# Four PSUM places for the transposes and one pair for the scores in the first batch of an attention and MLP kernel

## What is computed

```python
# attention, B, H, S, D = 4, 8, 576, 64
scores = causal_mask(q @ k.T / sqrt(D))
a = exp(scores - scores.max(-1)); a /= a.sum(-1) + 1e-9
phi = lambda x: where(x > 0, x, exp(x) - 1) + 1
mem = (phi(q) @ M_prev) / (phi(q) @ z_prev + 1e-6)
g = sigmoid(beta)                       # one gate for each head
x = g * mem + (1 - g) * (a @ v)         # 2304 tokens x 512
# first MLP, 512 -> 2048 -> 512
h = x @ w_in; y = (h * sigmoid(h)) @ w_out
# second MLP, 512 -> 1024 -> 512
h = y @ w2_in; u = h * softmax(h)
out = layer_norm(u) * g_ln @ w2_out
```

## Time and profile before

| | us |
|---|---|
| median of 3 runs | 880.93 |
| lowest and highest | 878.12, 881.41 |
| the profiled execution | 878.63 |
| its span, first to last instruction | 876.8 |

### The profile page before, as it was taken

The page is one execution under the profiler, slowest core; times in us unless marked ns, Lnnn a source line. Parts: engine busy times, 40 slices in busy tenths (PEclk is TensorE's granted clock), DMA queues, the critical chain, the costliest instruction groups (busy, mean ns, idle before and its releaser), DMA issues.

```text
span 876.8 us, 13106 instructions
## 1 busy us (share of the span) xinstructions
PE 834.5 (95%) x4576; PEld 702.8 (80%) x4576; DVE 524.0 (60%) x1003; ACT 405.3 (46%) x897; POOL 327.3 (37%) x350
## 2 busy tenths in 40 slices
PE   3868799999999999999999999999999999999998
PEld 2656677888788887878888879999998888888886
DVE  4787675876775576675575543144426666666664
ACT  3686676666655555565555434334121222222222
POOL 3667657677644455455544314133110000000000
PEclk9996789999999999999999999999999999999999
DMA  5222247657775454554444347333300000000000
GB/s 174 60 86 59 75 129 241 219 200 225 229 238 170 151 176 145 168 158 152 150 155 154 122 143 306 126 121 125 138 3 12 14 24 24 24 24 24 24 13 37
DMA packets 67480, 105.63 MB, mean 120 GB/s; under 512 B 29024, under 2 KB 40288, under 8 KB 67168
## 3 DMA queue, kind: packets, MB, share of 16 engines
q1 hardware_dynamic: 67120, 104.85, 36.7%
q10 hardware_dynamic: 304, 0.05, 0.0%
HBM read 83.38 MB, written 21.50 MB: 120 GB/s over the span
## 4 chain that ended last, share of the span: by engine, by line
PE 75%; DVE 5%; DMA 5%; SPq 4%; POOL 4%; ACT 4%; issue 2%; ACTq 0%
PE banks L1344 19%; PE banks L1332 18%; PE banks L1402 11%; PE banks L1463 11%; PE banks L1287 4%; PE banks L1309 4%; DMA wr_raw<-in_w_out 2%; PE banks L1249 2%; PE banks L1452 2%; SPq L493 2%; DMA z_row<-in_z_prev 1%; POOL vm L629 1%; PE banks L1303 1%; DVE pt_lo L984 1%; POOL g_lo L641 1%
## 5 line engine op out<-in xcount | busy, mean ns | idle before, releaser
L1344 PE MATMUL banks<-g_hi,wr 128*128 128x512 f32 (+1 forms) x640 | 197.2, 376 | 3.2 <-POOL g_lo L641 1.9
L624 POOL TENSOR_SCALAR prob<-prob,inv_sum,gate_all 128x576 f32<-128x576 f32 (+2 forms) x144 | 95.5, 674 | 106.9 <-DVE inv_sum L978 106.9
L1344 PEld LDWEIGHTS banks<-g_hi,wr 128*128 128x128 f32 x640 | 118.4, 188 | 18.9 <-issue 4.3
L1332 PE MATMUL banks<-xc_hi,wr 128*128 128x512 f32 x384 | 128.8, 402 | 0.0
L1344 PE MATMUL banks<-g_lo,wr 128*128 128x512 f32 (+1 forms) x320 | 117.6, 367 | 0.0
L984 DVE TENSOR_TENSOR pt_lo<-banks,pt_hi 128x512 fp32r<-128x512 f32 x144 | 83.7, 588 | 47.1 <-ACT pt_hi L721 46.2
L641 POOL TENSOR_TENSOR g_lo<-gu,g_hi 128x512 fp32r<-128x512 f32 x48 | 62.0, 1292 | 84.2 <-ACT g_hi L761 84.2
L715 ACT ACTIVATE prob<-banks,neg_max 128x576 f32<-128x576 f32 (+2 forms) x144 | 78.3, 548 | 30.0 <-DVE neg_max L970 26.9
L721 ACT ACTIVATE pt_hi<-banks 128x512 fp32r<-128x512 f32 x144 | 74.6, 520 | 34.4 <-PE banks L1287 31.4
L697 POOL TENSOR_TENSOR st<-st 128x1 f32<-128x1 f32 x18 | 9.9, 551 | 210.2 <-DVE st L1166 210.2
L1332 PEld LDWEIGHTS banks<-xc_hi,wr 128*128 128x128 f32 x384 | 72.9, 190 | 14.5
(11 more groups left out here) (126 smaller groups left out, 1785.4 us busy)
## 6 DMA issues: line engine op xcount, KB each, us to landing
wr<-split_w SPq DMA_DIRECT2D x96, 512.0 KB, 3.3
split_w<-wr SPq DMA_DIRECT2D x32, 512.0 KB, 4.5
k_raw<-in_k_t SPq DMA_DIRECT2D x16, 288.0 KB, 3.1
out<-o SPq DMA_DIRECT2D x18, 256.0 KB, 2.0
q_raw<-in_q_t SPq DMA_DIRECT2D x16, 256.0 KB, 2.7
vm_raw<-in_v_main SPq DMA_DIRECT2D x16, 256.0 KB, 2.5
wr_raw<-in_w_in SPq DMA_DIRECT2D x16, 256.0 KB, 3.8
wr_raw<-in_w_out SPq DMA_DIRECT2D x16, 256.0 KB, 3.7
```

What stands on the lines that cost most here:

```text
L624: pool.tensor_scalar(pr, pr, inv_sum[p % 2][:, columns(t, h)], gate, ALU.mult, ALU.mult).then_inc(prob_done, 1)
L1332: mm = pe.matmul(out_bank, w[:, a, k], x[:, k], start=(i == 0), stop=(i == 3 * KC - 1))
L1344: mm = pe.matmul(out_bank, w[:, a, k], g, start=(i == 0), stop=(i == 11))
```

## The change

In the first batch the turns take banks 2, 7, 5 and 6 one after the other, and the scores banks 0 and 1 alone. With it some instructions of the queues are moved: the four normalisations of tiles 1 and 0 come one step earlier, ahead of v_low, q_high comes one step later, at the end of ScalarE's step 2, one split of x comes one step later, and in the later batches the exponential of tile 0 comes one step earlier and q_low stands earlier in POOL's step.

```diff
@@ -39,8 +39,8 @@
 EXP_ALONE = [2, 2, 3, 5, 5, 7, 7, 8, 8]
-EXP_WOVEN = [1, 2, 2, 4, 4, 6, 7, 7, 8]
-SUM_ALONE = [3, 4, 6, 9]
+EXP_WOVEN = [1, 2, 2, 4, 4, 6, 7, 7, 7]
+SUM_ALONE = [3, 4, 6, 8]
 SUM_WOVEN = [3, 4, 6, 8]
@@ -58,10 +58,10 @@
-SCORES_ALONE = (0, 5)
+SCORES_ALONE = (0,)
 SCORES_WOVEN = 0
 
-TURN_ALONE = (2, 7)
+TURN_ALONE = (2, 7, 5, 6)
 TURN_WOVEN = (2, 7)
@@ -113,7 +113,7 @@
-X_BEFORE = [4, 2, 1, 1]
+X_BEFORE = [4, 1, 1, 1]
@@ -652,6 +652,9 @@ POOL, first batch
                 if pair_at(s, 4, 1):
                     q_low(pair_at(s, 4, 1))
+                for q, t in sums_of(s):
+                    for u, h in EXPS[EXPS.index((t, 0)):EXPS_AFTER[t]]:
+                        normalise(q, u, h)
                 if pair_at(s, -2):
                     phi_times_z(pair_at(s, -2))
...
                 if first_pass(s) is not None and MLP[first_pass(s)][0] == "H":
                     w_low(first_pass(s))
-                for q, t in sums_of(s):
-                    for u, h in EXPS[EXPS.index((t, 0)):EXPS_AFTER[t]]:
-                        normalise(q, u, h)
@@ -672,6 +672,8 @@ POOL, later batches
                     g_low(h_index(w[0], MLP[w[1]][1]))
+                if pair_at(s, 4, 1):
+                    q_low(pair_at(s, 4, 1))
...
                     w_low(first_pass(s))
-                if pair_at(s, 4, 1):
-                    q_low(pair_at(s, 4, 1))
@@ -813,8 +813,8 @@ ScalarE, first batch, and the same in the later batches
-                if pair_at(s, 1, 1):
-                    q_high(pair_at(s, 1, 1))
+                if pair_at(s, 2, 1):
+                    q_high(pair_at(s, 2, 1))
@@ -1058,18 +1058,18 @@ VectorE, first batch
                 if tile_of(s - 1):
                     row_max(*tile_of(s - 1))
+                for q, t in sums_of(s):
+                    sums(q, t)
                 if w and MLP[w[1]][0] == "H":
                     silu(h_index(w[0], MLP[w[1]][1]))
                 elif w and MLP[w[1]][1]:
                     add_y(w[0], *MLP[w[1]][1:])
-                for q, t in sums_of(s):
-                    sums(q, t)
                 if lows:
                     unit_lo(*lows[0])
+                if values_of(s - 1):
+                    add_half(*values_of(s - 1))
                 for q, u in lows[1:]:
                     unit_lo(q, u)
-                if values_of(s - 1):
-                    add_half(*values_of(s - 1))
```

## The result

The changed kernel takes 894.23 us in the median of four runs (891.9 to 895.37), the kernel before, measured beside it, 879.82 (878.12 to 881.41). The ratio is 1.0153, with a 95% interval from 1.0123 to 1.0182: slower by 1.5%, or 14.4 us, where 889 and +8.8 were forecast.

A forecast was written before the change was run, and what follows sets the result against it. Before 112 us a ring of waits between in-order queues bounds it, afterwards full TensorE. 4.6 + 0.8 + 1.5 + 2.5 - 0.6 = +8.8 us gives 887.4 on the profiled run, 889.7 on the median; forecast 889, range 882 to 896.

The forecast's parts named there:

- the late stage: From 112 us on TensorE is busy 408.8 of 411.9 us, so a later start moves the end equally.
- Part 1: Pair 0: with one pair of score banks, scores, maximum and exponentials run serially; +4.6 us, bounds 1.5 and 6.3.
- Parts 2 and 3: Later pairs: score waits and moved instructions cost +0.8 (pair 1), +1.5 (pair 2, full clock), +2.5 (pair 3, lower clock).
- rival (c): Longer idles bring the low clock into pairs 1 and 2, +3.3 us each; total 896; chance 0.12.
- Part 4: The rest: one split of x moves off the path to the last turn before the MLP, -0.6 us; other moves 0.
- the DMA strand: Pair 2: v_low behind the normalisations runs 1.05 us later, delaying the loads behind it and so phi_e.
- The four places: Four banks for the turns: their removed bank waits counted at nothing in steady pairs, within +0.1 in pair 0.
- (b): Only pair 0 pays, later score waits lying beside values and DMA: +4.0 us, 885; chance 0.15.
- (d): Faster: all 8.8 us of bank waits of the turns come back and later score waits hide; 876; chance 0.08.
- (e): The change does nothing that counts, since the late stage swallows it; chance 0.03.
- The rule cited before the result: First batch: cycling through PSUM banks leaves small idles that lower the clock; the time would be 896.

The follow-up runs named there:

- warm_after: Changed kernel plus matmuls of constants (fillers: 2, 5, 2, 6) ahead of the first batch's scores, into the next turn's bank: 879.67 us, ratio 1.0010.
- warm_before: Kernel before, banks and order unchanged, plus matmuls of constants (fillers) where TensorE waits in the first batch: 871.61 us, ratio 0.9909.
- warm_order: Changed kernel's moved instructions with the banks of the kernel before, plus the fillers of warm_before: 877.52 us, ratio 0.9958.
- two_places: Changed kernel with two banks (2, 7) for the turns in place of four: 892.94 us, ratio 1.0151.
- filled_one_pair: Kernel before with one pair of score banks in the first batch, plus matmuls of constants ahead of scores in pairs 1 to 4: 884.89 us, ratio 1.0061.
- warm_start: warm_before with more fillers in pair 0 where TensorE idles and fewer where it does not: 871.31 us, ratio 0.9908.

## Why the prediction was right or wrong

**What bounds it, and the late stage: right.** The end moved with the MLP's start, and the stage after it kept its length within 0.7 us.

**Part 1, pair 0, +4.6: right,** 26.45 against 21.85; that it is right to the decimal is luck, since 0.46 us of it is the earlier start of the first scores, and the end of the pair moved by 4.1. The scores of tile 3 start at 17.15 (forecast 17.1), those of tile 2 at 22.55 (22.4), the exponential of tile 2 at 25.24 (25.0).

**Parts 2 and 3, pairs 1 to 3, +0.8, +1.5 and +2.5: the chain's share right in the sum, the clock missed.** Measured 4.6, 5.9 and 1.7. At the full clock, warm_after against warm_before, pairs 1 to 3 differ by 2.2, 1.4 and 1.5 us, 5.1 together where I had 4.8. Only pair 2 is right by itself: pair 1 was put 1.4 too low, and pair 3 1.0 too high, from rows at a low clock, so that the sum agrees is partly luck. The step that failed is the assumption, in the heading of part 2, that pairs 1 and 2 stay at the full clock. They ran at 0.71 and 0.65. I had this as rival (c), and its price, 3.3 us a pair over the chain, gives 0.8 + 3.3 = 4.1 and 1.5 + 3.3 = 4.8 against 4.6 and 5.9; but I gave it 0.12, on the ground that the clock had held through pair 1. It had not quite: the column reads 1.00 there, but the matmuls up to 32.2 us take the low level's time (last section). The total of (c), 896, was too high by 2 and still nearer than my 889, which lay 5 too low. Pairs 1 and 2 came out above its price, pair 3 0.8 below, and pair 4 gained: 2.3 us shorter, at 0.85 where it had been at 0.71; and the kernel before, run beside the changed one, took 1.1 us less than the 880.93 that the sum started from.

**Part 4, -0.6: the step itself shows.** The last turn before the MLP, in the kernel before and in the changed one:

```profile
111.60 0.87 PE L1287 MATMUL banks<-ident,prob 128*128 128x128 f32 x3 [1.38 <-DVE pt_lo L984]
```

```profile
125.83 0.52 PE L1287 MATMUL banks<-ident,prob 128*128 128x128 f32 x3 [0.78 <-DVE pt_lo L984]
```

The wait is 0.6 shorter, but no run took the split of x by itself. With fillers pair 4 is 20.32 us in warm_after and 20.38 in warm_before, so at the full clock neither the 0.6 nor the rest of its gain is left.

**The parts of the schedule in part 2: half.** That v_low and the DMA strand would set phi_e 1.05 later did not show: v_low does run after the normalisations, from 36.15 in pair 1, but phi_e then waits for no load (48.85, above), because ScalarE came to it later than the load did. q_high does delay the second exponential of tile 3, which starts 0.75 after it; in pair 1 that cost nothing either, since the values ended at 43.67 and the scores of tile 2 at 44.26 found it done. Together the moves cost a little where there are two pairs of banks (1.5 us in warm_order's four windows), and there by another way than the forecast's: TensorE waits for v_low itself ahead of the values.

**The four places: right for this kernel.** They were counted at nothing beyond 0.1 in pair 0, and two_places shows 0.1 there and 0.4 in the sum. With fillers they are worth more (warm_after).

**Rivals.** (b), only pair 0 pays, falls with filled_one_pair, where pairs 1 to 3 still pay 1.8 to 2.7 each. (d), faster, falls with the result, and two_places shows why: the 8.8 us of bank waits were not on the path. (e) falls with the MLP's start.

**The split of the 14.45 us.** With the clock held from pair 1 on, the changed kernel's windows sum to 107.15 and those of the kernel before to 98.44, so 8.7 us are chain. That this is nearly the +8.8 of the forecast is chance in part, since that had other shares. The clock costs the kernel before 6.6 us and the changed one 12.4, and the difference is the other 5.7. With warm_start as the base the chain is 10.1 and the clock 4.4; the fillers of pair 0 decide which. The rule cited before the result, of the Trainium skill's "TensorE: Matmul & The Clock Gate", section "A second HAM failure mode: psum-queue depth-cycling", pointed the right way: the kernel that idles more behind its score banks lost more to the clock. The experiments add that it can be bought back with matmuls that do nothing.

## What to carry to other kernels

Idle time of TensorE that only stands beside another engine's chain was worth nothing here when a bank removed it. A chain that was two tiles wide and becomes one tile wide cost its whole round of scores, maximum and exponential in the first pair, 4 us and more, where nothing covers it, and 1.4 to 2.2 us in each later one. Where TensorE waits in every pair, price each pair at both clock levels before giving the low one a small chance. And where a stretch is bound by latencies, try matmuls of constants into a free bank ahead of TensorE's waits: here they gave 0.9% of the whole kernel, while none of the changes to the banks gave anything.

## What the runs showed of the hardware

The clock fell without a long pause. In pair 1 of the changed kernel it fell at about 36 us, within an idle time of 2.02 us that ended at 36.62. Windows of two microseconds, TensorE busy and granted clock:

```profile
32.00:34.00 2.00, 1.27 (x10) 1.00 0.01 2
34.00:36.00 2.00, 0.59 (x6) 1.00 0.00 0
36.00:38.00 2.00, 1.39 (x6) 0.54 0.00 0
```

In the profiles of warm_before and warm_order the fillers held it in seven of the eight pairs 1 to 4; in the eighth the mean was 0.85, so they lower the chance and are no guarantee.

The clock column reads 1.00 from the start of every profile, and is not to be believed there: the 288-column matmuls of pair 0 take 0.44 us each where those of pair 1 of the changed kernel take 0.29, under the same 1.00 (the first two rows below, both of the changed kernel). With early fillers, the column shows 0.78 for pair 0 (warm_before): it begins to tell once a change of level was recorded. So how long the start was slow has to be read from the matmuls. In the kernel before, the scores of tile 3 of pair 1 quicken between 32.20 and 32.62 us, 3.7 us after the pair began (the last two rows, the same form of matmul). That TensorE starts a program slow fits what the Trainium skill's "TensorE: Matmul & The Clock Gate" says in its part "The HAM clock gate", that the low level is the default and activity lifts it.

```profile
7.45 0.44 PE L1260 MATMUL banks<-k_hi,q_hi 128*128 128x288 f32 x1
...
33.52 0.29 PE L1260 MATMUL banks<-k_hi,q_hi 128*128 128x288 f32 x1
```

```profile
32.20 0.63 PE L1249 MATMUL banks<-k_hi,q_lo 64*128 64x512 f32 x2
32.62 0.47 PE L1249 MATMUL banks<-k_lo,q_hi 64*128 64x512 f32 x2
```

A small VectorE instruction may wait, and look busy, for as long as one of POOL's. In the changed kernel the addition of an epsilon to four numbers took 0.98 us and ended as POOL's phi_times_z did, at 33.9; in the three pairs behind it the same instruction takes 0.22, 0.22 and 0.44, and in the kernel before 0.16:

```profile
32.93 0.98 DVE L976 TENSOR_SCALAR inv_sum<-row_sum 128x4 f32<-128x4 f32 x1
```

```profile
32.34 1.55 POOL L610 TENSOR_TENSOR phi_by_z<-phi,z_row 128x640 f32<-128x640 f32 x1 [0.98 <-DVE phi L946]
```

No run here removed POOL's instruction, so the link is read from the two rows and not shown.
